# GpSimd's block loop in a routed feed-forward kernel: two nested loops, and the wait for the earlier scatter at the head of each block

## What is computed

```python
def _attn_ref(r, k, v, w, u):
    for t in range(S):
        cur = np.einsum('bhd,bhe->bhde', u[None] * kt, vt)
        y[:, :, t] = np.einsum('bhd,bhde->bhe', rt, state + cur)
        state = w[None, :, :, None] * state + np.einsum('bhd,bhe->bhde', kt, vt)

def _moe_ref(x, w_in, w_out):          # x [3072, 384], w_in [384, 2048]
    h = x @ w_in
    g = np.maximum(0.01 * h, h)
    return g @ w_out

def _moe2_ref(x, w_skip, w_gate, w1, w2):   # 8 experts, w1 [384, 1024], w2 [1024, 384]
    do_compute = x @ w_skip > 0
    out = x.copy()
    xc = x[do_compute]
    logits = xc @ w_gate
    e_idx = np.argmax(logits, axis=1)
    for e in range(E):
        mask = e_idx == e
        h = np.maximum(xc[mask] @ w1[e], 0.0)
        y[mask] = gate_w[mask, None] * (h @ w2[e])
    out[do_compute] = xc + y
```

## Time and profile before

| what | us |
|---|---|
| median of 3 runs (lowest, highest) | 673.41 (671.85, 675.17) |
| the profiled execution, its device time | 673.93 |
| its span in the trace | 672.2 |
| busy: PE, PEld, DVE, ACT, POOL | 645.7, 605.8, 402.0, 309.4, 82.6 |
| start of the last matmul, at L916 | 659.5 |
| start of the last scatter, at L1997 | 661.55 |

### The profile page before, as it was taken

The page is one execution under the profiler, slowest core; times in us unless marked ns, Lnnn a source line. Parts: engine busy times, 40 slices in busy tenths (PEclk is TensorE's granted clock), DMA queues, the critical chain, the costliest instruction groups (busy, mean ns, idle before and its releaser), DMA issues.

```text
span 672.2 us, 14206 instructions
## 1 busy us (share of the span) xinstructions
PE 645.7 (96%) x4733; PEld 605.8 (90%) x4734; DVE 402.0 (60%) x865; ACT 309.4 (46%) x682; POOL 82.6 (12%) x102
## 2 busy tenths in 40 slices
PE   7889999999999999999999999999999989999992
PEld 6779889999999999999999999999999879889982
DVE  7876666655656475466556545653466835956750
ACT  4465544444344443354334344433346336746740
POOL 4140000100010001001000100010021241233211
PEclk9999999999999999999999999999999999999997
DMA  8936625210422222242114221202406277694300
GB/s 216 292 131 210 210 70 175 73 56 25 139 68 72 69 86 67 64 142 72 44 33 138 72 72 40 67 8 81 185 1 212 83 246 267 208 352 155 120 21 8
DMA packets 39325, 78.09 MB, mean 116 GB/s; under 512 B 9032, under 2 KB 27494, under 8 KB 39216
## 3 DMA queue, kind: packets, MB, share of 16 engines
q1 hardware_dynamic: 34272, 62.96, 30.0%
q10 hardware_dynamic: 2432, 9.76, 4.2%
q0 software_dynamic: 2560, 4.58, 2.2%
HBM read 61.68 MB, written 13.00 MB: 111 GB/s over the span
## 4 chain that ended last, share of the span: by engine, by line
PE 86%; DVE 4%; ACT 3%; DMA 3%; issue 2%; ACTq 0%; POOL 0%; POOLq 0%; SPq 0%; DVEq 0%
PE bank L802 30%; PE bank L822 29%; PE bank L899 7%; PE bank L916 7%; PE bank L667 3%; PE bank L729 3%; DMA const<-in_consts 2%; PE bank L736 2%; PE bank L750 1%; PE bank L907 1%; ACT am L1086 1%; PE bank L856 1%; PE bank L892 1%; ACT wout_hi L1060 0%; DMA zg<-z_rows,get 0%
## 5 line engine op out<-in xcount | busy, mean ns | idle before, releaser
L1432 DVE TENSOR_TENSOR h_sb<-h_sb,bank 128x384 f32<-128x384 f32 x128 | 70.9, 554 | 158.9 <-ACT h_sb L1124 158.9
L1124 ACT ACTIVATE h_sb<-bank 128x384 f32<-128x384 f32 x128 | 62.8, 491 | 221.8 <-PE bank L802 221.5
L802 PE MATMUL bank<-x_hi,win_hi 128*128 128x384 f32 x384 | 135.0, 351 | 1.5 <-DVE win_lo L1477 0.9
L822 PE MATMUL bank<-wout_hi,g_hi 128*128 128x394 f32 x384 | 131.9, 343 | 1.5 <-DVE state L1408 1.5
L822 PE MATMUL bank<-wout_hi,g_lo 128*128 128x394 f32 x384 | 131.2, 342 | 0.0
L822 PE MATMUL bank<-wout_lo,g_hi 128*128 128x394 f32 x384 | 131.1, 341 | 0.0
L802 PE MATMUL bank<-x_hi,win_lo 128*128 128x384 f32 x384 | 129.4, 337 | 0.0
L802 PE MATMUL bank<-x_lo,win_hi 128*128 128x384 f32 x384 | 129.2, 336 | 0.0
L1439 DVE TENSOR_TENSOR g_lo<-h_sb,g_hi 128x384 fp32r<-128x384 f32 x128 | 71.7, 560 | 31.1 <-ACT g_hi L1131 30.1
L1131 ACT ACTIVATE g_hi<-h_sb 128x384 fp32r<-128x384 f32 x128 | 66.7, 521 | 46.1 <-DVE h_sb L1432 44.8
L802 PEld LDWEIGHTS bank<-x_hi,win_hi 128*128 128x128 f32 x384 | 72.1, 188 | 8.8 <-issue 6.3
(11 more groups left out here) (245 smaller groups left out, 890.4 us busy)
## 6 DMA issues: line engine op xcount, KB each, us to landing
raw<-in_experts SPq DMA_DIRECT2D x32, 768.0 KB, 6.2
rkt<-in_rk_t SPq DMA_DIRECT2D x46, 192.0 KB, 3.8
rkn<-in_rk_nat SPq DMA_DIRECT2D x21, 384.0 KB, 4.1
v<-in_v_nat SPq DMA_DIRECT2D x24, 192.0 KB, 3.0
z_rows<-z_sb SPq DMA_DIRECT2D x24, 192.0 KB, 2.9
out<-z_sb SPq DMA_DIRECT2D x24, 192.0 KB, 2.8
stage<-in_win ACTq DMA_DIRECT2D x4, 768.0 KB, 4.3
stage<-in_wout_t ACTq DMA_DIRECT2D x4, 768.0 KB, 6.2
```

The source lines that it names most:

```text
L802: mm = pe.matmul(h_ps[t % 2][:, 0:GT], a[:, kk, cols], b[G % 2][:, kk, :], start=n == 0, stop=n == 3 * KT - 1)
L822: mm = pe.matmul(z_ps[i][:, 0:ZW], a[t % 3][:, tok], b[:, f, :], start=f == 0 and j == 0, stop=f == FT - 1 and j == 2)
L1124: act.activation(h_sb[t % 2][:], h_ps[t % 2][:, 0:GT], ACT.Copy, scale=SLOPE).then_inc(s_h_scaled, 1)
L1432: dve.tensor_tensor(h_sb[t % 2][:], h_sb[t % 2][:], h_ps[t % 2][:, 0:GT], ALU.max).then_inc(s_leaky, 1)
```

## The change

It touches GpSimd's program alone. There are five edits:

1. The loop of 8 turns becomes two loops inside each other, of 2 parts with 4 turns each. An `If` on the part skips its four turns where none of them has a block. Block j is now block u of turn `4 * part + jj`.
2. The wait for the scatter of block 3 of a turn no longer stands at the end of that turn. Each block, u = 0 too, waits at its own head until the scatters before its own have landed, and frees a result buffer there.
3. The two scatters ahead of the loop count on `s_rows_out` as well, and the semaphore `s_rows_a_out` is gone. Every wait at a block's head counts 2 scatters more, and so block 0 waits for these two.
4. `s_res_free` starts at 1 in place of 2, because block 0 adds one at its head.
5. The end waits once, for `blocks` + 2 scatters.

```diff
-                    oob_is_err=False).then_inc(s_rows_a_out, 16)
+                    oob_is_err=False).then_inc(s_rows_out, 16)
...
-            pool.sem_inc(s_res_free, 2)
+            pool.sem_inc(s_res_free, 1)
...
-            with pool.Fori(0, (BLOCKS + 1) // UNROLL) as jj:
-                with pool.If(UNROLL * jj < blocks):
-                    for u in range(UNROLL):
-                        j = UNROLL * jj + u
-                        with pool.If(j < blocks):
-                            if u > 0:
-                                pool.wait_ge(s_rows_out, 16 * j)
-                                pool.sem_inc(s_res_free, 1)
...
-                            if u == UNROLL - 1:
-                                pool.wait_ge(s_rows_out, 16 * (j + 1))
-                                pool.sem_inc(s_res_free, 1)
-            pool.wait_ge(s_rows_out, 16 * blocks)
-            pool.wait_ge(s_rows_a_out, 16 * AHEAD)
+            def put_rows(j, u, turn):
+                pool.wait_ge(s_rows_out, 16 * (j + AHEAD))
+                pool.sem_inc(s_res_free, 1)
+                pool.tensor_copy(put[u % 2][:], id_put[:, bass.ds(spot_at(reg, j), 1)]).then_inc(s_ids_put, 1)
+                pool.wait_ge(s_ids_put, j + 1)
+                pool.sem_inc(s_pool_past, 1)
+                with pool.If(j < blocks - UNROLL):
+                    pool.wait_ge(rows_in[u], 16 * (turn + 1))
+                    pool.sem_inc(s_pool_past, 1)
+                    pick_ids(u, spot_at(far, j + UNROLL))
+                pool.wait_ge(s_res_done, j + 1)
+                pool.sem_inc(s_pool_past, 1)
+                pool.indirect_dma_start(
+                    out=out[:, :], out_offset=bass.IndirectOffsetOnAxis(ap=put[u % 2][:, 0:1], axis=0),
+                    in_=res[u % 2][:], in_offset=None, bounds_check=TOKENS - 1,
+                    oob_is_err=False).then_inc(s_rows_out, 16)
+                with pool.If(j < blocks - UNROLL):
+                    gather(u, j + UNROLL)
+
+            turns = (BLOCKS + 1) // UNROLL
+            with pool.Fori(0, 2) as part:
+                with pool.If(turns // 2 * UNROLL * part < blocks):
+                    with pool.Fori(0, turns // 2) as jj:
+                        with pool.If(turns // 2 * UNROLL * part + UNROLL * jj < blocks):
+                            for u in range(UNROLL):
+                                j = turns // 2 * UNROLL * part + UNROLL * jj + u
+                                with pool.If(j < blocks):
+                                    put_rows(j, u, turns // 2 * part + jj)
+            pool.wait_ge(s_rows_out, 16 * (blocks + AHEAD))
```

More of the change, by code:

```diff
@@ L373, in build @@
         s_res_a = sem("res_a")
-        s_rows_a_out = sem("rows_a_out")
         s_spots = sem("spots")
```

## The result

The change measured 670.18 us (median of 9 runs, 668.91 to 672.55) against 672.67 us for the kernel before on the same chip (median of 9). The ratio is 0.9959, with a 95% interval of 0.9943 to 0.9976: 2.8 us less, between 1.6 and 3.8. The ratio compares the means of the nine runs; the medians are 2.5 us apart. The forecast was 670.0 us and 3.4 us less. That the time itself came within 0.2 us of it is in part luck: the forecast started from a median of 673.41 us, and the kernel before measured 0.7 us less than that over nine runs. The gain is the number to judge it by.

The account below looks back on a forecast made before the run. PE bounds the kernel to about 660 us, but the span's last 8 us are GpSimd's alone: empty turns and drain. From 673.9, -3.4 + 0 + 0 gives 670.5, or 670.0 us against the median; range 668.2 to 673.8.

Parts of the forecast that it names:

- The term of the sum: Program's end: with the wait moved and loops nested, GpSimd's last wait passes at 664.0 instead of 667.4, 3.4 us less.
- the empty turns: GpSimd's five loop turns holding no block, behind the last scatter's landing: 0.6 us each by the trace.
- The loops' end under the landing: After the last scatter's issue, the remaining loop instructions finish at 663.3, hidden by its landing at 664.0, 0.7 us to spare.
- Six pairs: Loop tests and branches left after the last scatter, counted as instruction pairs: 0.29 us a pair, 1.7 us in all.
- The drain: GpSimd's DRAIN at the program's end: taken as 4.32 us from its own start, wherever it starts.
- The rival that it takes the gain back: GpSimd's final drain ends by something the last scatter began, lasting 7.8 us from 664.1; span unchanged, 673.4; chance 0.17.
- The half-lost case: GpSimd's loops' end is longer, for instance by one 1.7 us code stop; gain 2.4 us, time 671.0; chance 0.12.
- the slower rival: Five jumps at GpSimd's program end each fetch code, 1.7 us each; 4.4 us lost, 677.8; chance 0.04.
- What was costed at nothing: Block 0's new wait and the earlier copies of blocks 4 and 8 fall in GpSimd's idle time: zero each.
- The wait at block 0: Block 0's head: two copies end by some 558.2, the scatter stays at 561.10, over 2 us left; zero.
- The copies of blocks 4 and 8: At these blocks' heads branches run during the scatter; copies come some 0.5 us earlier, scatters still wait for DVE; zero.

Follow-up runs that it names:

- one scatter ahead waited for: The change, but block 0 waits at its head only for the first of the two scatters ahead of the loop, the second at the end; ratio 0.9946.
- the waits alone: Kernel before with the change's waits at each block's head, but still one loop of 8 turns; ratio 0.9961, 2.6 us less.
- the change with drains: The change plus one more GpSimd drain in each block, ahead of its wait for DVE's result; 665.38 us, ratio 0.9883.
- the kernel before with drains: Kernel before plus one more GpSimd drain in each block, ahead of its wait for DVE's result, nothing of the change; ratio 0.9944.

## Why the prediction was right

**The term of the sum.** 3.4 us less was forecast from the empty turns, and the distance from the last scatter to the end shrank by 3.4 us. The device time gave 2.8, with an interval up to 3.8 that holds 3.4. The kernel that ends in the same way, with one scatter ahead waited for, gave 3.6, and in the table rows and device time are never more than 0.6 us apart, to either side. In the traces no version lost more than 0.4 us between the first copy into `get` and the last scatter, and the change lost 0.2. The rest of the 0.6 us is found nowhere in the changed part, so I take it for scatter of the runs. One source of it is seen: the stretch of half the granted clock in the first 22 us. Of the nine runs of the change the five with a mean granted clock of 0.995 to 0.997 took 668.9 to 670.9 us, the four at 0.992 and 0.993 took 670.2 to 672.6. How many of the nine runs before had such a stretch isn't on record, so that it makes up the 0.6 us isn't shown.

**The loops' end under the landing.** Six pairs at 0.29 us were to be over 1.7 us behind L2004's place, with 0.7 us of the landing to spare. They took 1.5 us (663.1 to 664.6), and the wait passed 1.0 us later, at the landing. The run with the waits alone shows the same price where it isn't covered.

**The drain.** It was taken as 4.32 us from its own start, and it took 4.324. The rival that it takes the gain back is refuted: it began 3.4 us sooner behind the scatter and was no longer. The reason that I gave, that GpSimd has nothing left over from a transfer, was wrong, though. There is something left over, 0.083 us for each transfer, which only a drain pays, while a copy behind a gather starts at once. The number was right because the change leaves the number of transfers at 52; no row that the prediction read showed that this is what counts, so here it was lucky. The drain at the start of the program had no transfer before it; its 0.19 us are more than the 0.03 to 0.05 of the other drains without one, and what it waited for isn't shown. By the Trainium skill ("PSUM — Partial Sum Buffer", section Engine vs sequencer instructions) a drain waits until the engine is fully idle. The drain over two multiplications agrees, 2.66 us until they were done.

**The half-lost case and the slower rival.** Both lived on code that has to be fetched. The loops' end took 1.5 us with no stop in it, and the table of DMA queues has the same 25 and 36 instruction transfers before and after:

```profile
q8 instruction: 36, 0.59, 0.4%
q14 instruction: 25, 0.20, 0.1%
```

The Trainium skill ("Runtime: NRT & Kernel Launch", section Instruction fetch mechanics) warns of a stall where a taken branch leaves the two pages that are held; no stall shows at these jumps. An estimate of what the longer jump costs in place of a fetch, from the two kinds of empty turns, is 0.07 us: (0.61 - 0.47) / 2, if the length is the cause. In the case *Slower* the prediction says that two such fetches "only use up the gain"; by its own numbers they leave 0.7 us of it (3.4 - 3.4 + 0.7), which changes no chance.

**What was costed at nothing.** The wait at block 0 was to move two copies to about 557 and leave the scatter at 561. The first of them came at 558.1 and the scatter at 562.7, or 556.6 and 561.2 with the 1.5 us of the later start taken off. PE's waits at the blocks' first products and their transposes were to stay within 1 us: after, in the list of who waited for whom from 530 us,

```profile
PE bank L898 <- DVE zt_lo L1817: 1.4, 2, 1.2
PE bank L891 <- DMA zg<-z_rows,get: 1.3, 1, 1.3
```

against 1.2 before for the second and, for the first,

```profile
PE bank L899 <- DVE zt_lo L1818: 1.3, 2, 1.1
```

The copies of blocks 4 and 8 were to come some 0.5 us earlier. From the wait's passing to the copy it was 1.2 us before in both (596.0 to 597.2, 633.0 to 634.2) and is 0.6 after (598.3 to 598.9, 634.9 to 635.6). Their scatters start no earlier for it, as was forecast.

## What to carry to other kernels

Read the end of a trace on the sequencers' lines, not only in the chain of work: here 8 of the last 10 us belonged to an engine that the profile called 12% busy, in a loop that had nothing left to do and in a drain. A wait that stands ahead of such work makes it serial with the transfer; moved behind it, the work is free as far as the transfer covers it, here 2.5 us of the 3.2. And where GpSimd issues many indirect transfers, put drains where it idles: the price of the last one goes with the number of transfers since the one before. A drain put there also waits for transfers that are still under way, so look at what stands behind it.

## What the runs showed of the hardware

- GpSimd's drain cost 0.04 us and 0.083 us for each indirect transfer of 128 rows since the last drain: 0.03 to 0.05 us for none, 0.12 for 1, 0.22 for 2, 0.29 for 3, 3.57 for 43, 4.32 for 52.
- Where transfers were under way, it also lasted until they had landed: 2.42 us behind a single scatter that took 2.5 us to land; 3.19 us in block 6 of the change with drains, to 0.1 us behind a gather's landing; 7.7 us in block 0 of the kernel before with drains, to 1.4 us behind the landing of the second scatter ahead. What the 1.4 us are isn't shown.
- With 52 transfers it took 4.32 us both when it began behind the landing and when it began 1.0 us ahead of it.
- A turn of a loop with nothing to do cost GpSimd's sequencer 0.22 us without an `If`, 0.47 with one over a short body, and 0.61 over the code of four blocks.
- TensorE's granted clock was at 1.2 GHz for some 6.8 us between 14 and 22 us in the profiled execution of the change, behind 4 us in which PE was busy for 2.6, and at 2.4 GHz in the same stretch of that of the kernel before. By 130 us the first was 1.3 us behind.
